# Two-mixer transformer block on one core: the first mixer's early weight entries are read as plain fp32 sums and split in the ring

## The reference

```python
q_s = exp(q - max(q, -1));  q_s = q_s / (sum(q_s, -1) + 1e-9)      # softmax over head_dim
k_s = exp(k - max(k, 2));   k_s = k_s / (sum(k_s, 2) + 1e-9)       # softmax over the sequence
attn = einsum('bhsd,bhde->bhse', q_s, einsum('bhsd,bhse->bhde', k_s, v))   # 8 batches, 8 heads, 576, 64
x  = attn as (8, 576, 512)
u  = x + (relu(x.T @ w_tok1) @ w_tok2).T                           # tokens 576 -> 256 -> 576
y  = u + relu(u @ w_ch1) @ w_ch2                                   # first mixer:  512 -> 1536 -> 512
xn = (y - mean(y)) / sqrt(var(y) + 1e-6) * g_ln
out = y + relu(xn @ w_ch1') @ w_ch2'                               # second mixer: 512 -> 2048 -> 512
```

## Time and profile before

| | us |
|---|---|
| runs | 1562.66, 1572.3, 1573.31 |
| profiled execution: time | 1563.69 |
| profiled execution: span | 1561.9 |
| PE busy | 1472.2 (94%) |
| DVE, ACT, POOL busy | 1076.6, 698.2, 309.0 |

### The profile page before, as it was taken

How to read it: one execution, slowest core, us unless ns; L and a number is a source line. 1 busy time by engine, 2 the same in 40 slices (tenths; PEclk the granted TensorE clock), 3 DMA queues, 4 the chain that set the end, 5 groups by cost and what they waited for, 6 DMA issues and landing times.

```text
span 1561.9 us, 19837 instructions
## 1 busy us (share of the span) xinstructions
PE 1472.2 (94%) x7584; PEld 1322.4 (85%) x7584; DVE 1076.6 (69%) x1165; ACT 698.2 (45%) x844; POOL 309.0 (20%) x315
## 2 busy tenths in 40 slices
PE   6999896898999999899989999999999999999998
PEld 5988885787888887788878888888888888889998
DVE  7987876397486486496696687568657856872276
ACT  5656654352453453352452453344345424532342
POOL 6587785323303312300000000000000000000000
PEclk9999998899999999999999999999999999999999
DMA  7899985989989989979658767766876687667766
GB/s 241 256 306 296 299 282 202 403 318 366 354 291 379 372 294 362 352 288 317 240 184 300 248 209 266 249 247 219 275 243 228 237 277 244 211 219 256 251 214 199
DMA packets 150334, 429.28 MB, mean 275 GB/s; under 512 B 14240, under 2 KB 43488, under 8 KB 150240
## 3 DMA queue, kind: packets, MB, share of 16 engines
q1 hardware_dynamic: 132768, 361.94, 67.6%
q0 software_dynamic: 17472, 66.07, 11.8%
HBM read 348.26 MB, written 79.69 MB: 274 GB/s over the span
## 4 chain that ended last, share of the span: by engine, by line
PE 74%; DMA 10%; DVE 7%; issue 3%; SPq 2%; POOL 2%; ACT 2%; DVEq 0%; ACTq 0%; POOLq 0%
PE ps L1131 24%; PE ps L1133 23%; PE ps L1132 23%; DMA w_ring<-w_scratch_B 6%; DMA vt<-v 2%; SPq L289 2%; DMA qt<-q 1%; DVE o_lo L980 1%; DVE x_lo L834 1%; PE ps L1155 1%; DMA w_op<-w2b 1%; PE ps L1166 1%; DVE q_sum L761 1%; POOL q_lo L464 0%; DVE h L950 0%
## 5 line engine op out<-in xcount | busy, mean ns | idle before, releaser
L1131 PE MATMUL ps<-x_hi,w_ring 128*128 128x462 f32 (+1 forms) x980 | 369.2, 377 | 44.1 <-issue 15.1
L1131 PE MATMUL ps<-o_hi,w_ring 128*128 128x462 f32 (+1 forms) x980 | 367.4, 375 | 9.6 <-DVE o_lo L980 7.9
L1133 PE MATMUL ps<-x_hi,w_ring 128*128 128x462 f32 (+1 forms) x980 | 366.7, 374 | 0.0
L1132 PE MATMUL ps<-x_lo,w_ring 128*128 128x462 f32 (+1 forms) x980 | 366.7, 374 | 0.0
L1132 PE MATMUL ps<-o_lo,w_ring 128*128 128x462 f32 (+1 forms) x980 | 364.8, 372 | 0.0
L1133 PE MATMUL ps<-o_hi,w_ring 128*128 128x462 f32 (+1 forms) x980 | 364.6, 372 | 0.0
L671 ACT CAST o_hi<-h 128x924 fp32r<-128x924 f32 (+1 forms) x210 | 202.3, 963 | 254.8 <-PE ps L1133 225.0
L980 DVE TENSOR_TENSOR o_lo<-h,o_hi 128x924 fp32r<-128x924 f32 (+1 forms) x210 | 240.8, 1150 | 61.2 <-ACT o_hi L671 61.2
L1131 PEld LDWEIGHTS ps<-x_hi,w_ring 128*128 128x128 f32 x980 | 186.2, 190 | 74.3 <-issue 31.2
L1131 PEld LDWEIGHTS ps<-o_hi,w_ring 128*128 128x128 f32 x980 | 185.1, 189 | 40.1 <-issue 17.5
L950 DVE TENSOR_TENSOR h<-ps,h 128x924 f32<-128x924 f32 (+1 forms) x90 | 100.6, 1117 | 163.5 <-PE ps L1133 163.1
(11 more groups left out here) (140 smaller groups left out, 1831.3 us busy)
## 6 DMA issues: line engine op xcount, KB each, us to landing
w_ring<-w_scratch_C SPq DMA_DIRECT2D x280, 512.0 KB, 3.8
w_ring<-w_scratch_B SPq DMA_DIRECT2D x210, 512.0 KB, 5.6
w_scratch_C<-w_out POOLq DMA_DIRECT2D x8, 1792.0 KB, 11.7
w_scratch_C<-last_pair POOLq DMA_DIRECT2D x8, 1792.0 KB, 11.8
w_scratch_B<-w_out POOLq DMA_DIRECT2D x6, 1792.0 KB, 10.4
w_scratch_B<-last_pair POOLq DMA_DIRECT2D x6, 1792.0 KB, 9.9
kt<-kT SPq DMA_DIRECT2D x32, 288.0 KB, 6.0
u_scratch<-u_out SPq DMA_DIRECT2D x32, 288.0 KB, 3.8
```

Of the source, the lines that this page charges most:

```text
L1131: mm(dst, a_hi, b_hi, start=start, stop=False, skip_group_check=onto)
L1132: mm(dst, a_hi, b_lo, start=False, stop=False, skip_group_check=onto)
L1133: return mm(dst, a_lo, b_hi, start=False, stop=stop, skip_group_check=onto)
```

## The change

1. In stage B the entries of calls j = 0 and j = 1 (14 of 42 in each position, 70 in all) are not stored as hi and lo but as plain fp32 sums: units 0 to 3 get no `hi_unit` and `lo_unit`, POOL stores the seven sums (`store_sums`, 896 KB) from `w_op` into `w_sums_B`, and SP loads an entry of 256 KB into the lo half of its ring slot. ACT then makes hi in the ring (`hi_entry`), DVE makes lo in place (`lo_entry`), and PE waits for `wr_lo` in place of `w_in`. They do it at the start of entry n - 2's part (`SPLIT_AT`), for entries 0 to 3 at the end of phase A.
2. `UNITS_A` is 6: units 6 and 7 are loaded and summed at the end of phase A, but their hi and lo move into phase B. `HI_AT` is now 2, 4, 9, 11, 15, 17 for units 6 to 11 (before 2, 5, 8, 12 for 8 to 11) and 28, 37 for 12 and 13 (before 27, 36). POOL's loop is now: load unit n + 2, store unit n, sum unit n + 2.
3. The splits of the first tokens (`hi_x`, `lo_x`, `sum_x` of position 0) move earlier, into step 7.
4. `vt` has its column of ones between two blocks of 128 channels; the host lays the values out by partition, and v comes in five other DMAs: one with runs of 256 floats (1,024 bytes; 128 × 7), four with 512-byte runs.

```diff
-    UNITS_A = NB
-    HI_AT = {e: UNITS_A + i for i, e in enumerate((2, 5, 8, 12, 27, 36))}
+    UNITS_A = NB - 2
+    HI_AT = {e: UNITS_A + i for i, e in enumerate((2, 4, 9, 11, 15, 17, 28, 37))}
+    def plain(stage, j):
+        return stage in "B" and 0 <= j < G1S[stage] - 1
+    PLAIN = [c.e0 + p for c in CALLS if plain(c.stage, c.j) for p in range(7)]
+    for n in PLAIN:
+        if n >= RW:
+            first = [c.e0 for c in CALLS if c.e0 <= n and (c.j == 0 or c.j < 0)][-1]
+            SPLIT_AT[max(n - 2, first - 1)].append(n)
...
             def load_v(b):
                 wait(sp, kv_done, b)
-                for t, rows in ST:
-                    sp.dma_start(vt[0:rows, t, :, 0:P], v[b, t * P:t * P + rows, :].rearrange("p (c e) -> p c e", c=NC))\
-                      .then_inc(v_in, 16)
+                full = vt[:, 0:NT - 1, :, :].rearrange("p t a w -> p (t a w)")
+                w, n = 2 * P + 1, (NT - 1) * NC // 2
+                src = v[b, 0:P * n * 2 * P].rearrange("(p x) -> p x", p=P)
+                sp.dma_start(full[:, P + 1:P + 1 + (n - 1) * w].rearrange("p (n w) -> p n w", w=w)[:, :, 0:2 * P],
+                             src[:, P:P + (n - 1) * 2 * P].rearrange("p (n w) -> p n w", w=2 * P)).then_inc(v_in, 16)
...
+                if n in TURN:
+                    sp.dma_start(w_ring[:, n % RW, :, 1, :].bitcast(fp32), wp_dram[c.stage][local])\
+                      .then_inc(w_in[n % RW], 16)
+                    return
...
+            def store_sums(n):
+                stage, j, k, e = where(n)
+                pool.wait_ge(wp_sum, 4 * (n + 1))
+                pool.dma_start(wp_dram[stage][7 * j:7 * j + 7, :, k, :].rearrange("q p f -> p q f"),
+                               w_op[:, n % 2, 0:7, :]).then_inc(wp_sums_stored[n % 2], 16)
...
             batches(step)
-            load_unit(NB)
-            sum_unit(NB - 1)
-            lo_unit(NB - 1)
-            store_unit(NB - 1)
-            for n in range(NB, U0["C"] + UNITS["C"]):
-                sum_unit(n)
-                if n + 1 < U0["C"] + UNITS["C"]:
-                    load_unit(n + 1)
-                store_unit(n)
+            sum_unit(UNITS_A + 1)
+            for n in range(UNITS_A, U0["C"] + UNITS["C"]):
+                if n + 2 < U0["C"] + UNITS["C"]:
+                    load_unit(n + 2)
+                if split_unit(n):
+                    store_unit(n)
+                if n + 2 < U0["C"] + UNITS["C"]:
+                    sum_unit(n + 2)
...
+            def hi_entry(n):
+                act.wait_ge(w_in[n % RW], 16 * (n // RW + 1))
+                nc.scalar.copy(w_ring[:, n % RW, :, 0, :], w_ring[:, n % RW, :, 1, :].bitcast(fp32)).then_inc(wr_hi, 1)
...
+            def lo_entry(n):
+                x = w_ring[:, n % RW, :, :, :]
+                dve.wait_ge(wr_hi, TURN[n] + 1)
+                nc.vector.tensor_tensor(x[:, :, 1, :], x[:, :, 1, :].bitcast(fp32), x[:, :, 0, :], ALU.subtract)\
+                  .then_inc(wr_lo, 1)
...
                     if later == 0 and c == 0:
-                        inputs_over(dve)
-                        lo_x(0, 0)
+                        lo_x(0, 2)
+                        sum_x(0, 2)
                 if later == 0:
-                    lo_x(0, 1)
-                    sum_x(0, 1)
-                    lo_x(0, 2)
-                    sum_x(0, 2)
                     lo_x(0, 3)
+                    lo_entry(2)
+                    lo_entry(3)
                     lo_x(0, 4)
```

More of the change, by code:

```diff
@@ L624, in step @@
                             hi_q(i + 1, ST[c - 1:c])
-                    if later == 0 and c == 0:
-                        hi_x(0, 1)
+                    if later == 0 and c == 1:
+                        hi_x(0, 2)
+                        hi_x(0, 3)
+                    if later == 0 and c == 2:
+                        hi_x(0, 4)
                 if later:
                     hi_q(i + 1, ST[3:])
-                if later and not first:
+                if later and not first and split_unit(i - 1):
                     hi_unit(i - 1)
@@ L691, in norm @@
                       .then_inc(root_made, 1)
-            hi_unit(NB - 2)
-            for p in (2, 3):
+            hi_entry(2)
+            hi_entry(3)
+            for p in (5, 6):
                 hi_x(0, p)
-            hi_unit(NB - 1)
             for c in CALLS:
@@ L700, in _ @@
                     for p in range(7):
+                        for n in SPLIT_AT[c.e0 + p]:
+                            hi_entry(n)
                         if p in (0, 1, 2, 6):
                             take(c, p)
-                        if c.index == 0 and p < 3:
-                            hi_x(0, 4 + p)
                         if p == 4:
@@ L724, in _ @@
                             hi_o(c, n // c.epp, n % c.epp)
-                        if c.e0 + n in HI_AT:
+                        for m in SPLIT_AT[c.e0 + n]:
+                            hi_entry(m)
+                        if c.e0 + n in HI_AT and split_unit(HI_AT[c.e0 + n]):
                             hi_unit(HI_AT[c.e0 + n])
@@ L885, in step @@
                     max_q(i + 1, ST[3:])
+                if later == 0:
+                    sum_x(0, 1)
+                    lo_entry(0)
+                    lo_entry(1)
                 for c in range(NC):
@@ L1069, in _ @@
                     for p in range(7):
+                        for n in SPLIT_AT[c.e0 + p]:
+                            lo_entry(n)
                         if p == 0 and c.j > 0:
@@ L1074, in _ @@
                         for part in range(2):
-                            if c.e0 + p - 1 - part in HI_AT:
+                            if c.e0 + p - 1 - part in HI_AT and split_unit(HI_AT[c.e0 + p - 1 - part]):
                                 lo_unit(HI_AT[c.e0 + p - 1 - part], part)
@@ L1105, in _ @@
                             relu_t1(CALLS[c.index - 1])
+                        for m in SPLIT_AT[c.e0 + n]:
+                            lo_entry(m)
                         for part in range(2):
-                            if c.e0 + n - 1 - part in HI_AT:
+                            if c.e0 + n - 1 - part in HI_AT and split_unit(HI_AT[c.e0 + n - 1 - part]):
                                 lo_unit(HI_AT[c.e0 + n - 1 - part], part)
@@ L1339, in tokens_first @@
         return np.ascontiguousarray(a.transpose(0, 2, 1, 3)).reshape(B, S, C)
+    values = tokens_first(inputs["v"])
+    full = values[:, 0:S // 128 * 128]
     arrays = {
```

100 lines of the change are left out of this document (72 added, 28 removed).

## The result

| | before | after |
|---|---|---|
| median of 4 runs (us) | 1567.5 | 1581.0 |
| lowest and highest | 1562.3 to 1573.3 | 1580.0 to 1585.3 |
| profiled execution: span | 1561.9 | 1579.2 |

The ratio after to before is 1.0099, with an interval of 1.0067 to 1.013: slower by 1%, where 1554 us was forecast. The same kernel, run again later, gave 1.0084 (1.0059 to 1.0108).

The account below looks back on a forecast made before the run. It took PE's waits for v in phase A and for late ACT and ring loads early in phase B as the bound. Terms -8 - 3.5 + 1.5 - 2.5 - 1 took 1563.7 to 1550.2, plus 4: 1554 us, range 1539 to 1574.

Parts of the forecast that it names:

- What bounds the kernel, phase A: Phase A: quicker v loads and halved stores remove PE's waits for v; -8 us, bounds -11 and -3.
- The start of phase B: Entries 0 to 23: two large waits go, a chain of unit loads and sums becomes the bound; -3.5 us.
- rival A: Start of phase B: unit loads land fast, in 5 us, giving back 10 us; 1543 us, chance 0.16.
- the sum: Whole kernel: the forecast's worked-out times added up, -13.5 us on the profiled 1563.7, giving 1550.2 us.
- +1.5: Behind the wait at entry 23: matmuls at 1.2 GHz after some 10 us idle cost about 1.5 us.
- The rest of the first position: Position 0 after entry 23: part of 5.2 us of PE idle goes; -2.5 us, 0 to -5.
- Positions 1 to 4: 56 plain entries: halved loads against a landing deadline of 6.0 us, mostly even; -1 us, -8 to +25.
- C: Positions 1 to 4: plain entries arrive late, each delaying its successor; 1592 us at a landing of 8.0, chance 0.08.
- Two bounds of the prediction: Positions 1 to 4: over 1% slower from landing 7.6; start of phase B: landing 10, store 13 give +20 us.
- The base: Whole kernel before: profiled 1563.7 us, plus 4, half of the 8.6 by which the median of runs lay above.
- B: Phase A stays as long, waits for v becoming waits for lo of q and DVE; 1561 us, chance 0.19.
- D: Start of phase B: unit loads land in 13.3 us in most cycles, 31 us more; 1585 us, chance 0.05.

Follow-up runs that it names:

- e4: The kernel before with only the new layout and loads of v; ratio 1.0013 to the kernel before.
- e3: The kernel after without plain entries, all units stored as hi and lo; 1575.0 us, ratio 1.0038 to the kernel before.
- e2: The kernel after with POOL's old order of sum, load, store; 1572.5 us, ratio 1.0025 to the kernel before.
- e13: The kernel after with POOL's old order and no plain entries; ratio 0.9998 to the kernel before.
- e14: The kernel after with POOL's old order and plain entries loaded but not split in positions 1 to 4; ratio 0.9954 to the kernel before.
- e1: The kernel after with plain entries loaded but not split in positions 1 to 4; 1570.6 us, ratio 1.0024 to the kernel before.
- e8: The kernel after with POOL's units taken in pairs and no plain entries; ratio 1.0002 to the kernel before.
- e15: The kernel after with each plain entry loaded twice, splits kept; 1610.9 us, ratio 1.029 to the kernel before.

## Why the prediction was wrong

**What bounds the kernel, phase A: right.** -8 was forecast; it ended 5.8 us sooner, in a second pair of executions 11.0 us. The waits for v fell to 2.2 us, and what is late next is what I named, the lo of q at 4.9. Both parts that I named gave something: of v's own layout e4 shows 3.3 us, of the halved stores e3 shows 5. The section "Why small descriptors are slow" of the page "DMA: Bandwidth & Descriptors" of the Trainium skill gives, as an estimate, at most 8% for v, some 2 us over six steps. The waits for v in e4 fell by 4.6 us, but SP's five issues of v also took 6.1 us there (80 to 100) and 9.1 before; no run tells the packets from the issues.

**The start of phase B: the mechanism right, two terms off.** The first take (2.9 us forecast as 3.3), the loss of both large waits, the sums each behind its load, the last ring load behind store 11 and the half clock behind it came as worked out. The wait at entry 23 was 7.3 us for some 10. The second loads landed in 5.2 us in the median and not in 7.0, nearly rival A's 5, which should have won 10 us. It did not, because of two terms. The four sums of a unit took 3.9 to 5.3 us and not the 2.9 of the earlier trace rows, 8.5 us more in five units; what made them slower no run tested, but DVE was busy for 70 of the 106 us of this stretch and for 59 of 100 before. And POOL stood 3.8 us for the lo of unit 8, for which the sum had nothing. So a unit took 11.8 us and not 10.65. For entries 0 to 23 the sum has 329.4 - 243.5 = 85.9 us (its +1.5 lies behind entry 23); it took 93.2 and 90.9.

**The rest of the first position**: -2.5 was forecast, and the +1.5 belongs here. From entry 23 to the end it took 385.8 - 330.8 = 55.0 us, against 387.0 - 332.9 = 54.1 before: no gain, a miss of 1.9.

**Positions 1 to 4: the step that failed.** "A plain load must land in 6.0 us ... Mostly even: -1". The deadline was right and the price was taken at the wrong loads. I compared it with a typical landing, and the typical one is indeed 3.3 us. But a landing counts where it is longest: behind a unit's load and store (2.36 MB, at the 401 GB/s of 500 to 505 an estimated 5.9 us of traffic), a quarter of the plain loads took 6.5 to 10.8 us. At the starts of positions 2 and 3 such a load had 7.6 us before and cost PE 1.7 and 1.3; now it had 6.0, came behind a unit's load as well as its store, and cost 4.1 and 4.8, and each of these two waits was followed by matmuls at 1.2 GHz. Two things follow which I had not put in the sum. The order of POOL was priced at the start of phase B alone, though it holds for every unit of stage C too: it costs 6 to 12 us in all, and in the profiled executions 6 to 15 in positions 1 to 4 (e2, e13 and e14 against after, e3 and e1). At these two loads alone the order shows little: in e2, with the old one, they landed in 10.8 and 9.1 us and cost 3.7 and 3.1. And the clock after a wait was priced at one place (+1.5), while here it made PE busy 10 us longer in the first pair of executions, and 2 in the second. Against the forecast of -1 stood +13 to +19.

**The rivals.** C named the right place, the right deadline and the right sign; its price was in the form of a steady landing L in all entries, whose condition (a median of 7.6) did not come true, and a chance of 0.08 rested on that. B and D did not happen, A's landings nearly did, without A's gain. Two bounds of the prediction do not come out of their terms, and nothing hangs on either: by C's formula 1588 us takes a landing of 7.8 and not 7.6, and a landing of 10 with a store of 13 gives +16.5 and not +20. The base was right: 1567.7 for a kernel of before in a typical run (1563.7 + 4), and the later medians were 1565.9 to 1568.1. The profiled execution took 1581.2 us against 1550.2 of the sum. Of these 31 us, 19.5 are positions 1 to 4, 7.3 are entries 0 to 23, 1.9 the rest of position 0 and 2.2 phase A; the 4 us on top of the sum make it a miss of 27 against the forecast.

**What stays open.** Why v's 3.3 us in phase A do not show in the time of e4, whose positions 1 to 4 took 464.0 us against 457.4 and 462.4 of before. Positions 1 and 2 are hit hard and 3 is not; POOL issues nothing from 715 to 760, around the end of position 3, which fits, but no run moved a unit there. Why one wait is followed by the slow clock and another is not. A version that beats both kernels was not found: e8 and e13 are even with before. e14, which leaves the splits out, shows what halved bytes would bring if the splits were free: half a per cent.

## What to carry to other kernels

When a load gets a processing step behind it, price the shorter deadline at the slowest loads of the stretch, not at the median: look up which transfers go out just ahead of them, and what a wait costs with the slow clock behind it. A change in the order of issues on one queue holds for every round of its loop; cost it in each stage, and ask of a buffer both when it is filled and when its store lets it go. Fewer bytes gave less here (2 to 7 us, known to some 6) than two short steps added between landing and use cost (9 to 12 us), though the engines that did them had room.

## What the runs showed of the hardware

Loads of one size and one queue, 256 KB, landed in 2.9 to 10.8 us in one stretch, with a median of 3.3. The first load of position 2, 256 KB in after and 512 KB in e3, both behind a unit's load and store, landed in 10.2 and 10.5 us, that of position 3 in 10.8 and 13.4: three times the median, and the traffic issued in the few microseconds ahead did more to it than the size. Loading each of them twice, bytes and issues both doubled, lengthened the kernel by 30 us (e15).

After a wait of 4.13 us the granted clock was 0.54 in its window, and for thirteen matmuls it cost, beyond the wait itself, 0.18 us each. Not every such wait does this. After the 3.48 us at entry 42 of before the matmuls started 0.21 us apart at a clock of 1.00 (386.9 to 390.3). In the second execution of before only 1.92 us stood ahead of a stretch at 0.50 (622.9 to 626.2):

```profile
622.60 0.50 PE L1131 MATMUL ps<-x_hi,w_ring 128*128 128x462 f32 x1 [1.92 <-issue]
622.89 0.59 PE L1132 MATMUL ps<-x_lo,w_ring 128*128 128x462 f32 x1
623.28 0.59 PE L1133 MATMUL ps<-x_hi,w_ring 128*128 128x462 f32 x1
```
